# Chain steps spread evenly over the tiles, and experts in 25 whole and six half slots, in a fused attention and mixture-of-experts kernel

## The reference

```python
def _attn_ref(q, k, v, a_re, a_im):              # (4, 8, 768, 48)
    mag = np.sqrt(a_re * a_re + a_im * a_im)
    scale = np.minimum(mag, 0.999) / (mag + 1e-06)
    ...
    for t in range(S):                           # complex state per head, 48 x 48
        S_re, S_im = (ar * S_re - ai * S_im + kv, ar * S_im + ai * S_re)
        y[:, :, t] = np.einsum('bhd,bhde->bhe', q[:, :, t], S_re)
def _moe_ref(x, w_in, w_out, g_ln):              # x (3072, 384), w_in (384, 1024)
    h = x @ w_in
    solu = h * softmax(h)
    ln = (solu - mu) / np.sqrt(var + 1e-06) * g_ln
    return ln @ w_out
def _moe2_ref(x, w_gate, w_noise, noise, w1, w2):    # 8 experts, (384, 1024), (1024, 384)
    noisy_logits = x @ w_gate + log1p(exp(x @ w_noise)) * noise
    top2, top2_w = ...                           # the two best experts of each row, softmaxed
    for e in range(E):
        for k in range(2):
            mask = top2[:, k] == e
            out[mask] += top2_w[mask, k, None] * (np.maximum(x[mask] @ w1[e], 0.0) @ w2[e])
```

## Time and profile before

| | |
|---|---|
| runs | 1185.85, 1188.84, 1189.65 us (median 1188.84) |
| profiled execution | 1187.08 us |
| its span | 1185.3 us |
| mean granted clock of TensorE | 0.939 |
| PE, DVE, ACT, POOL busy | 89%, 73%, 55%, 39% of the span |
| first phase | to about 611 us |
| slots | 628.3 to 1173.6 us |

### The profile page before, as it was taken

How to read it: one execution, slowest core, us unless ns; L and a number is a source line. 1 busy time by engine, 2 the same in 40 slices (tenths; PEclk the granted TensorE clock), 3 DMA queues, 4 the chain that set the end, 5 groups by cost and what they waited for, 6 DMA issues and landing times.

```text
span 1185.3 us, 21982 instructions
## 1 busy us (share of the span) xinstructions
PE 1051.0 (89%) x7898; PEld 987.8 (83%) x7898; DVE 866.0 (73%) x1592; ACT 646.7 (55%) x1105; POOL 457.6 (39%) x413
## 2 busy tenths in 40 slices
PE   0456898898898899999948999999999999999996
PEld 0245787897797798978838999999999999999995
DVE  5789889888889988645544767777776676676672
ACT  7734675664765745645524555555555555555551
POOL 4011133254354343434522543543443453454342
PEclk9867899898899899999968999999999999999998
DMA  9430121121230211111306767767667676676640
GB/s 262 149 97 24 41 88 53 42 88 39 57 88 31 65 35 54 48 55 35 128 10 239 245 201 266 251 213 256 227 239 258 234 240 226 227 259 209 227 145 1
DMA packets 85980, 167.51 MB, mean 141 GB/s; under 512 B 18566, under 2 KB 57696, under 8 KB 85872
## 3 DMA queue, kind: packets, MB, share of 16 engines
q1 hardware_dynamic: 72336, 137.61, 36.3%
q0 software_dynamic: 13440, 28.40, 6.5%
q10 hardware_dynamic: 96, 0.10, 0.0%
HBM read 148.83 MB, written 21.92 MB: 144 GB/s over the span
## 4 chain that ended last, share of the span: by engine, by line
PE 60%; DVE 3%; issue 2%; ACT 2%; DMA 1%; POOL 0%; POOLq 0%; DVEq 0%; ACTq 0%; SPq 0%
PE bank L1415 23%; PE bank L1612 22%; PE bank L1476 4%; PE bank L1524 4%; PE bank L1406 3%; PE bank L1498 2%; PE bank L1536 1%; ACT z L942 1%; PE bank L1542 0%; DVE turn L1041 0%; PE bank L1556 0%; PE bank L1513 0%; PE bank L1452 0%; DVE zl L1250 0%; DVE w1l L1140 0%
## 5 line engine op out<-in xcount | busy, mean ns | idle before, releaser
L970 ACT ACTIVATE hh<-bank 128x256 fp32r<-128x256 f32 x248 | 95.3, 384 | 255.1 <-PE bank L1415 255.1
L1415 PE MATMUL bank<-sxh,w1h 128*128 128x256 f32 x744 | 211.9, 285 | 2.1 <-DVE sxl L1365 2.1
L1415 PE MATMUL bank<-sxh,w1l 128*128 128x256 f32 x744 | 210.1, 282 | 0.0
L1415 PE MATMUL bank<-sxl,w1h 128*128 128x256 f32 x744 | 209.8, 282 | 0.0
L1384 DVE SCALAR_TENSOR_TENSOR hl<-bank,hh 128x256 fp32r<-128x256 f32 x248 | 105.0, 423 | 119.5 <-ACT hh L970 106.4
L695 POOL DMA_INDIRECT out<-yo,mine x62 | 77.5, 1250 | 277.9 <-DVE yo L1377 260.0
L1612 PE MATMUL bank<-w2h,hh 128*128 128x384 f32 x496 | 167.0, 337 | 0.0
L1612 PE MATMUL bank<-w2l,hh 128*128 128x384 f32 x496 | 166.4, 336 | 0.0
L1612 PE MATMUL bank<-w2h,hl 128*128 128x384 f32 x496 | 166.2, 335 | 0.0
L1415 PEld LDWEIGHTS bank<-sxh,w1h 128*128 128x128 f32 x744 | 140.6, 189 | 2.5 <-DVE sxl L1365 2.5
L1415 PEld LDWEIGHTS bank<-sxh,w1l 128*128 128x128 f32 x744 | 141.3, 190 | 0.0
(11 more groups left out here) (202 smaller groups left out, 2397.1 us busy)
## 6 DMA issues: line engine op xcount, KB each, us to landing
raw<-in_w SPq DMA_DIRECT2D x62, 1536.0 KB
ar<-in_a_re SPq DMA_DIRECT2D x6, 768.0 KB, 4.6
turn<-in_a_im SPq DMA_DIRECT2D x6, 768.0 KB, 6.5
qk<-in_q SPq DMA_DIRECT2D x48, 96.0 KB, 2.4
qk<-in_k SPq DMA_DIRECT2D x48, 96.0 KB, 2.5
out<-wide SPq DMA_DIRECT2D x9, 512.0 KB, 11.7
vt<-in_v SPq DMA_DIRECT2D x24, 192.0 KB, 2.6
xs<-x SPq DMA_DIRECT2D x24, 192.0 KB, 2.7
```

The lines of the kernel that those rows point to most:

```text
L970: nc.scalar.activation(hh[:, f % NH, :], bank[:, f % 2, 0:CAP], ACT.Relu).then_inc(hh_done, 1)
L1415: ins = MM(dst, stationary[a_](cc), moving[b_](cc), start=(n_ == 0), stop=(n_ == len(terms) - 1))
```

## The change

It has these parts.

1. The chain steps. `PRODUCTS` gives way to `FILLS`, which gives for each tile of a round the steps in each of seven places of DVE's body. With c > 0 the tiles get 22, 20, 19 and 2 steps (before 12, 28, 17 and 6), with c = 0 they get 0, 16, 34 and 13 (before 0, 20, 33 and 10). No steps lie inside the gate any more.
2. The order beside them. On ACT `inverse_squares(2c + 2)` goes ahead of the logs of the fourth tile, `inverse(2c + 2)` behind xh, and in tile 1 the logs to the end of the body. On DVE `norm(2c + 5)` goes from the end of the body to a place ahead of the reciprocal, and in tile 2 `norm(4)` behind z.
3. The slots. 25 whole slots of 256 rows and six half slots of 128 (numbers 5, 10, 15, 20, 25 and 30); the slot table has 24 steps. In a half slot the hidden product has the tokens stationary: two parts of nine matmuls of 512 columns of w1, which give h by rows. ACT copies them to `row_h`, PE turns them (eight transposes), ACT and DVE make hh and hl of four blocks at a time, and the result takes 24 matmuls of 384 columns. Three pieces of w1 of the slot after a half slot are split at the end of the slot before it.
4. raw1 and raw2 have two buffers each, and loads are issued a slot earlier.
5. On POOL the output rows of slot s are gathered ahead of the tokens of slot s + 2, and after a half slot `give` on DVE moves to a later block (`give_block`: 4 for the half slot, 3 and 2 for the next two).

```diff
-SLOTS = (2 * NTOK - (E - 1)) // CAP + E
+WHOLE, HALVES = 25, 6
+SLOTS = WHOLE + HALVES
+HALF_SLOTS = (5, 10, 15, 20, 25, 30)
...
+def give_block(s):
+
+    return max([GIVE] + [4 - (s - t) for t in HALF_SLOTS if t <= s])
...
-        PRODUCTS = ((0, 20, 53, 63), (12, 40, 57, 63))
+        FILLS = (((0, 0, 0, 0, 0, 0, 0), (0, 0, 0, 0, 0, 0, 16), (4, 1, 6, 1, 2, 12, 8), (13, 0, 0, 0, 0, 0, 0)),
+                 ((6, 1, 7, 1, 2, 5, 0), (12, 1, 3, 1, 2, 1, 0), (9, 1, 4, 1, 2, 2, 0), (2, 0, 0, 0, 0, 0, 0)))
...
             def load_w1(s):
-                e = sp.value_load(slot_expert[0:1, bass.ds(s, 1)], min_val=0, max_val=E - 1)
-                apart(sp, (w1_lo, KC * s))
-                sp.dma_start(raw1[:], w1[bass.ds(e, 1)].rearrange("e (c p) f -> p (e c) f", p=P)).then_inc(raw1_loaded, 16)
+                e = sp.value_load(slot_expert[0:1, bass.ds(table_row(s), 1)], min_val=0, max_val=E - 1)
+                apart(sp, (w1_lo, KC * (s - 1)))
+                sp.dma_start(raw1[s % 2][:], w1[bass.ds(e, 1)].rearrange("e (c p) f -> p (e c) f", p=P)).then_inc(raw1_loaded[s % 2], 16)
...
             for s in range(SLOTS):
+                partial(s, s % 2, s % NM)
                 if s + 2 < SLOTS:
                     gather(s + 2, s % 2, (s + 2) % NM)
-                partial(s, s % 2, s % NM)
                 give(s, s % 2, s % NM)
...
+                if b == 3 and prep:
+                    inverse_squares(2 * c + 2)
                 if b == 3 and ahead:
                     logs(2 * c + 5)
...
-                if b == 1 and ahead:
+                if b == 1 and 0 < c < C - 2:
                     logs(2 * c + 4)
...
-                if b == 3 and prep:
-                    inverse_squares(2 * c + 2)
-                    inverse_squares(2 * c + 3)
                 if b == 3 and ahead:
                     scale(2 * c + 5)
+                if b == 3 and prep:
+                    inverse_squares(2 * c + 3)
...
-                if b == 3 and prep:
-                    inverse(2 * c + 2)
...
                     nc.scalar.activation(xh[0:PR].rearrange("p c t -> p (c t)"), bank[0:PR, 7, :], ACT.Copy).then_inc(xt_hi, 1)
+                if b == 3 and prep:
+                    inverse(2 * c + 2)
...
+                if first_one:
+                    logs(2 * c + 4)
```

ACT's program of a half slot:

```diff
+            def half_slot(s, par, more):
+
+                s0, k = steps(s), 2 * HALF_SLOTS.index(s)
+
+                def row(part):
+                    act.wait_ge(h2_mm, s0 + part + 1)
+                    wait(act, row_turned, k - 1 + part)
+                    nc.scalar.activation(row_h[:, 512 * part:512 * (part + 1)], bank[:, part, :], ACT.Relu).then_inc(row_done, 1)
+
+                def high(part):
+                    act.wait_ge(row_turned, k + part + 1)
+                    act.wait_ge(y2_mm, s0 - 2 + 2 * part)
+                    nc.scalar.activation(hh_half[:, 4 * part:4 * (part + 1), :].rearrange("p k t -> p (k t)"),
+                                         bank[:, turn_bank(par, part), :], ACT.Copy).then_inc(hh_done, 1)
+
+                row(0)
+                if more:
+                    tokens(s + 1, 1 - par)
+                row(1)
+                high(0)
+                high(1)
+                if more:
+                    for j_ in range(W2P):
+                        w2_piece(s + 1, 1 - par, j_)
```

DVE's body of a tile, where `fill(k)` does the steps of place k:

```diff
-                if b == 2 and c + 2 < C:
+                if b == 2 and 0 < c < C - 2:
                     norm(2 * c + 4)
-                if not waiting:
-                    fill(2)
+                if b == 3:
+                    fill(0)
                 if n <= T:
                     gate()
-                if not waiting:
-                    fill((4, 10, 5, share)[b])
+                if b < 3:
+                    fill(0)
...
                 if b == 3 and prep:
                     state_decays(c + 1)
-                if not first_one:
-                    fill(3)
+                if b == 3 and c + 2 < C:
+                    norm(2 * c + 5)
+                fill(2)
```

PE's program of a half slot:

```diff
+            def half_slot(s, par, more):
+
+                if more:
+                    tokens(s + 1, 1 - par)
+                half_hidden(s, par, 1)
+                half_turn(s, par, 0)
+                half_turn(s, par, 1)
+                if more:
+                    first_hidden(s + 1, 1 - par)
+                half_result(s, par, 0)
+                half_result(s, par, 1)
```

More of the change, by code:

```diff
@@ L51, with is_half, table_row, units @@
 LN_LIMIT = math.log(0.999)
+def is_half(s):
+    return s in HALF_SLOTS
+def table_row(s):
+    return WHOLE + HALF_SLOTS.index(s) if is_half(s) else s - sum(t < s for t in HALF_SLOTS)
+def units(s):
+    return 1 if is_half(s) else SUB
+def units_upto(s, step=1):
+    return sum(units(t) for t in range(s, -1, -step))
+def give_block(s):
+    return max([GIVE] + [4 - (s - t) for t in HALF_SLOTS if t <= s])
+def steps(s):
+    return sum(2 if is_half(t) else FC for t in range(s))
 def wait(eng, sem, value):
@@ L1194, in body, with fill @@
                 prep = c + 1 < C
-                share = PRODUCTS[c > 0][b] if prep else 0
-                made = [PRODUCTS[c > 0][b - 1] if prep and b else 0]
-                first_one = c == 0 and b == 1
-                waiting = first_one
-                def fill(count=1):
-                    for k_ in range(made[0], min(share, made[0] + count)):
-                        product_op(c + 1, k_)
-                        made[0] = k_ + 1
+                fills = FILLS[c > 0][b] if prep else (0,) * 7
+                made = [sum(map(sum, FILLS[c > 0][:b]))]
+                def fill(place):
+                    for k_ in range(fills[place]):
+                        product_op(c + 1, made[0] + k_)
+                    made[0] += fills[place]
                 def gate():
@@ L1222, in gate @@
                             V.max(top[:, t], nl[:, 1, t]).then_inc(gate_step, 1)
-                        fill(not waiting)
                         apart(dve, (gate_step, s0 + 2 + count))
@@ L1307, in body @@
                     k_products(n)
-                if b == 3 and c + 2 < C:
-                    norm(2 * c + 5)
-                if not first_one:
-                    fill(10)
+                fill(5)
                 if has(m):
@@ L1360, in _ @@
-            then(V.tensor_copy(tail_row[:], rank_base[one]))
+            for i_ in range(2):
+                then(V.tensor_tensor(fills[:, i_], count.unsqueeze(2).to_broadcast([P, E, MAXS]), thresh[:, i_], ALU.is_gt))
+            then(V.tensor_reduce(cnt[:, 1:3, :], fills[:], AX.X, ALU.add))
+            then(V.tensor_tensor(odd, any_, whole, ALU.subtract))
+            then(V.tensor_tensor_scan(pairs_upto, ones[:, 0:E], whole, 0.0, ALU.mult, ALU.add))
+            then(V.tensor_tensor_scan(odd_upto, ones[:, 0:E], odd, 0.0, ALU.mult, ALU.add))
@@ new lines, in _ @@
+            then(V.tensor_tensor(odd_ahead, odd_upto, odd, ALU.subtract))
+            in_pairs, in_odd = (slot_cmp[:, i_] for i_ in range(2))
+            own = in_pairs
+            at_pair, at_odd = (x[:].unsqueeze(2).to_broadcast(by_slot) for x in (pair_no, odd_no))
+            then(V.tensor_tensor(in_pairs, over(pairs_upto), at_pair, ALU.is_le))
+            then(V.tensor_reduce(slot_f[:, 0, :], in_pairs, AX.X, ALU.add))
+            then(V.tensor_tensor(in_pairs, in_pairs, over(whole), ALU.mult))
```

287 lines of the change are left out of this document (189 added, 98 removed).

## The result

The changed kernel takes 1182.32 us (median of 12 runs, 1176.31 to 1186.79) beside 1189.57 us for the kernel before (12 runs, 1185.85 to 1192.95). The ratio is 0.9944, 95% interval 0.9928 to 0.9961: 7 us gained where 69 were forecast. The profiled execution took 1186.79 us (span 1185.1), against 1187.08 (span 1185.3) before.

A forecast was written before the change was run, and what follows sets the result against it. PE was taken to bound the slots; in the first phase, uneven DVE work and ACT's order left PE holes. Terms 24 + 45 - 2.5 + 1.9 = 68.4 us off 1188.84 gave 1120 us, range 1108 to 1149.

The forecast's parts named there:

- first phase: Rounds of four tiles before the slots: evened chain steps and ACT's new order gain 2.5 + 20 + 1.7 = 24 us.
- POOL's order: Output rows gathered ahead of tokens in the slots: tokens 0.5 us late at five places, 2.5 us lost.
- landed: End of POOL's gather chain in a slot: token gathers land 2.2 us after their issue, scatters after 1.9.
- Half slots: Six half slots of 10.3 us each, less 0.3 for fewer transposes, against a 17.56 us period: 45 us saved.
- Cost nothing: ACT and DVE around a half slot: at most 24.4 us of work fits in 27.9 us, no loss.
- cost nothing by itself: Weight loads issued a slot earlier into two raw buffers: same traffic, DMA share 0.65 to 0.71, no cost.
- norm ahead of the reciprocal: In tile 11 on DVE, the norm waits for ACT's scale ahead of the reciprocal: 1 us added.
- move of ScalarE's squares: Fourth tile on ACT: two squares go ahead of the logs, taking 1.6 us from in front of L931.
- rival (1): First phase: evening does nothing, the hole moves to tile 8's end; 27 us lost, 1147 us; chance 0.17.
- (2): Slots: token gathers late around half slots, two loads in flight; 3 us at ten places, 30 us, 1150; chance 0.13.
- (3): Slots: ACT or DVE hold a half slot as long as a whole one, 44 us back, 1164 us; chance 0.04.
- (4): Slots: slower than before, each gather 4.0 us or more late with half clock behind, up to 1217 us; chance 0.03.

The follow-up runs named there:

- order_back: The changed kernel with the token rows for two slots on gathered ahead of the output rows again, as before the change: 1148.6 us, ratio 0.9658.
- experiment 3: Weight loads of slots 2 to 30 cut to a third of w1 and a quarter of w2: changed kernel 1152.57 us, order_back 1136.66 us.
- no_halves: order_back with 31 whole slots in place of 25 whole and six half ones: 1182.02 us, ratio 0.9920.
- gates_back: The changed kernel with the weight loads gated as late as before the change, two raw buffers kept: 1208.38 us, ratio 1.0187.
- Experiment 5: First-phase steps moved singly and together; for the third tile's norm, order_back with it moved behind the tile's first product steps: 1138.60 us, ratio 0.9557.
- three_back: order_back with fourth tile's norm behind the k products, inverse squares behind the exponential, third tile's norm behind its first product steps: 1135.38 us, ratio 0.9539.

## Why the prediction was wrong, point by point

The forecast was 1120 us. The measured way from there to 1182.3 has three pieces: first phase 19 (first tokens at 619.6 in place of 600.7), order 33.7, and some 9 that order_back is still behind, for slow landing behind half slots (12 by experiment 3, 11 by its ratios, of which the sum held 2.5).

- **POOL's order: the step that failed.** The sum gave it 2.5 us, bounds 0 and 3 at ten places; it cost 34. Its chain was right to 0.3 us up to the last issue. The term "landed" was mis-sized: 2.2 us from the end of the issue, where slot 5 shows 5.3; from the start of the issue it is 3.2 against a median of 6.0. The 2.2 came from the slots' first gather (621.50 to 624.74), before which no weight load had been issued since 562.75; the next went out at 622.83. The scatter's 1.9 came from the tail as well, behind the last load (1139.62). With 0.5 us to spare, the landing was the number that mattered. The text did say that no row shows a landing beside the loads, and then priced it from the row nearest in kind, not in circumstances. The trace did hold the circumstances. In a slot of the kernel before the second token gather is issued at 675.43, 1.0 us behind a load, and over its flight the DMA engines' share is not the stage's 0.65 but 1.01:

```profile
675.43:681.90 6.47, 6.47 (x48) 6.47 (x47) 4.91 (x8) 4.13 (x8) 3.44 (x3) 1.00 1.01 351
```

Its landing is in no view, but the updates of its semaphore put it at 6.5 us, and the median of the second token gather over 31 slots at 6.3. Nothing waited for it there. The Trainium skill, "DMA: Bandwidth & Descriptors", section "Anatomy of one DMA — SWDGE (gpsimd) path", gives a fit with no term for other traffic; worked out for such a transfer, an estimate, it is 2.45 us. The best landings here (2.1 to 2.8 us) agree with it, the median beside loads (6.0) doesn't.
- **A third of the places was missed.** The bound counted ten places, the half slot's start and the slot behind it; a third wait stands in the slot after that (1.16 us at 757.48), 15 in all. GpSimd's lag is carried over from slot to slot. And behind each longer hole TensorE runs at a lower clock, which the sum didn't price for this step.
- **Half slots: right.** 10.0 us each against 10.3 less 0.3, 0.25 us for row_h against 0.45, and 47.1 us with the tail against 46.9, once rows land fast. "Cost nothing" for VectorE around them was wrong by the same landing: with full loads it waits for output rows (21.2 us in order_back), and TensorE waits 7.1 us for low pieces behind it. Half slots were worth 5.6 us each and not 7.56.
- **Loads "cost nothing by itself": right in one sense only.** Two buffers and early loads cost nothing (no_halves) and are needed with rows first (gates_back). But a load is what the gathers share the DMA engines with, and the price was put on the mean share, 0.65 to 0.71, which hides stretches at 1.01.
- **First phase: 24 forecast, 5 measured.** Tiles 8 and 9 came as computed, to 0.2 us. Three terms failed. The norm ahead of the reciprocal was priced at 1 us, on the ground that ScalarE reads z late; but VectorE stood still for 3.48 us, and the state add, the k products and xl queue behind it. It is a small term by itself (2.3 us). The move of ScalarE's squares was counted only as a gain of 1.6 us in front of the copy of x2. What they wait for at their new place, VectorE's last carry, was never asked: 13.3 us in the first round, 2.5 in the others, with the scores and the exponential queued behind (6.6 us in all). The third tile's norm was priced as busy time. In the kernel before it waits for nothing: ScalarE's magnitude is begun at 269.64, ahead of the tile's xl (270.13), and the norm stands at 273.07. With tile 9 cut from 23.6 to 18.9 us, xl comes at 267.31 and the magnitude, behind its chain on ScalarE and GpSimd, only at 271.75; the norm waits 2.3 us. Experiment 5 gives 6.4 us for it, of which 2.7 lie in its own tiles. The rest, 8.4 us, has the price that rival (1) named, steps beside GpSimd at two to four times their cost alone, not in tile 8 but in tile 10; that is read from one tile's trace and wasn't tried by an edit.
- **The rivals.** (2) came true near its price, 34 us against 30, though at 15 places. It was argued down by "today's prev gathers run beside loads, with a wait of 1.9 at most"; that 1.9 is GpSimd's wait for a scatter ahead of the gather, and says nothing of the gather's own landing. Its cause, two loads in flight together, wasn't tested apart from one load. (1) came near in size (19 of its 27 us) and not in mechanism: tile 8 lasts as computed, and 11.2 us of the loss are the three moved steps. The rivals were weighed one at a time, so that the range ended at 1149. They lie in different phases and exclude nothing; together they give 1120 + 27 + 30 = 1177, which is near 1182 in part by luck, as (1) was right for another reason. (3) fell. (4) didn't come about: the landing is 3.1 us longer than taken, not 4.0.
- **What would show it** named the right sign ("if PE waits for xg by several us").

## What to carry to other kernels

Here a gather's landing went with what else the DMA engines carried at that moment, so a chain with little to spare must be priced with the landing under load. Where no view shows one because nothing waited for it, read the DMA share over the few us of the flight and not over the stage, and take the time of the load beside it as a first bound. If a step is moved on an engine that works in program order, ask first what it waits for at its new place, then who stands behind it. And where two things that can go wrong lie in different stages, add them: the range must hold both.

## What the runs showed of the hardware

- A gather of 128 rows of 1.5 KB lands 2.1 to 2.8 us after the start of its issue at best. In the median the output rows' took 4.3 us beside small loads (113 GB/s) and 6.2 to 6.6 beside full ones (221 to 239 GB/s, mean share of the DMA engines 0.63 to 0.69); the token gathers took 6.0 with rows first and 3.6 to 3.7 with tokens first. So the stage's mean traffic doesn't tell it; the share during the flight does better. In three_back, of 93 gathers of the slots whose landing the trace gives, the 32 that flew at a share of 0.9 or more took 6.6 us in the median (5.4 to 8.3), and the 21 at less than 0.5 took 3.2 (2.2 to 4.2).
- A VectorE step of two SBUF operands took up to four times as long beside a GpSimd step (1.47 us against 0.35), and the next one, right behind that GpSimd step, took 0.35 again.
- The changed kernel's times spread by 10.5 us (12 runs), those of order_back by 5.3 (4 runs) and of three_back by 2.6 (4 runs). But the kernel before, whose chain isn't late, spread by 11.8 us in one set (17 runs), so the spread is no sign of a late chain.
